# Squared-relu attention and a gated feed-forward: matmuls over all 128 rows replaced by pairs over 64 rows, in steps of two tiles

## The chip, the cores and the metric

The kernel runs on one core of a Trainium2 chip (trn2). The metric is device time in microseconds (us) of one execution, as the median of several. The engines are called by their short names: PE (TensorE, matmuls; PEld are its weight loads), DVE (VectorE), ACT (ScalarE), POOL (GpSimd) and SP (SyncE, which issues the DMAs). SBUF is the on-chip memory that all of them read, PSUM the eight banks that PE writes.

## The reference

Four batches of 3136 positions go through an attention without softmax and then a gated feed-forward with a convolution of three taps over positions. Inputs and outputs are float32.

```python
scores = (1 / S) * (z @ z.T)                 # S = 3136, z is 3136 x 64
x = u * (np.maximum(scores, 0) ** 2 @ v)     # u and v are 3136 x 256
h = np.maximum(x @ w_in, 0)                  # 3136 x 1024
conv = sum(conv_w[k] * shifted(h, k - 1) for k in range(3))
out = (h / (1 + np.exp(-conv))) @ w_out      # 3136 x 256
```

## The kernel before

Everything is held transposed, so that positions of a query lie along the free axis. The work is cut into 28 **blocks** of 448 query positions, seven to a batch. For each block the keys are walked in 25 **tiles** of 128 rows (the last has 64). Matmul operands are float32r; to keep precision each operand is split by ACT and DVE (or POOL) into a rounded part (`_hi`) and a remainder (`_lo`), and a product is the sum of three matmuls: hi by lo, hi by hi and lo by hi. A matmul takes weights of 128 rows by 128 columns and streams 448 columns (450 in the block that closes a batch).

For a tile `j` of block `n` the steps are these:

- `scores` (PE, L276 to L291): two matmuls into one bank of `ps_s`. z has only 64 features, so hi and lo parts lie one above the other in the 128 rows of `z_st`, and two matmuls give the whole product.
- ACT writes the scaled relu (`relu_s`, L422); DVE multiplies it by the scores in the bank (L563, `attn`), which gives the squared relu. For every two tiles ACT rounds (`attn_hi`, L417) and DVE takes the remainder (`attn_lo`, L551).
- `attend` (PE, L293 to L315): three matmuls for each of the two halves `c` of the 256 columns of v, into the two banks of `ps_av`.

After the last tile DVE multiplies `ps_av` by u (`x_sb`, L577). The feed-forward of block `n - 1` is done while block `n` is attended: for each of eight tiles `f` of the 1024 hidden columns `up` (six matmuls into `ps_h`), relu on ACT (`h_sb`, L454), first tap on ACT (L464), second and third on DVE (L590, L598), sigmoid on ACT (L470), the gate product on DVE (L604), rounding on ACT (`g_hi`, L476), the remainder on DVE (`g_lo`, L610, which raises `gated_split`), and for each pair `F` of hidden tiles `down` (twelve matmuls into `ps_y`, L345, which waits for `gated_split`).

Each engine has its own instruction queue, written in program order. A step of the loop is one tile: `scores` run `LEAD = 5` tiles ahead of `attend`, with three banks for scores. Two tables say in which step after its `up` each stage of the feed-forward is written on its engine:

```python
START = (3, 6, 10, 14)
STAGE = {"relu": 1, "tap0": 1, "tap1": 3, "tap2": 4, "gate": 5, "gated": 5, "round": 7, "split": 7, "down": 10}
```

So a split of pair `F` stands in step `START[F] + 7` and the `down` that reads it in step `START[F] + 10`, three tiles later. In the last block's feed-forward, with no attention beside it, other tables (`_ALONE`) hold. At the end of each batch ACT and POOL also round and split the next batch's z and v piece by piece (`z_st`, `v_hi`, `v_lo`).

## Time and profile before

| | |
|---|---|
| median of 3 runs | 1732.62 us (1732.59 to 1732.87) |
| profiled execution, its own time | 1733.34 us |
| its span, first to last instruction | 1731.6 us |
| PE busy | 1690.8 us (98%), 8232 matmuls and as many weight loads |
| DVE, ACT, POOL busy | 1370.7, 1217.3 and 196.0 us (79%, 70%, 11%) |
| share of the chain that ended last | PE 87%, DVE 5%, ACT 3% |
| mean granted PE clock | 0.996 |

The busy time of PE adds the time in which at least one matmul was under way; since one matmul is recorded for 0.36 us while the next starts 0.20 us later, it doesn't tell how close PE is to its rate. For that the distance from start to start is read from the timeline or from the counts in a window.

### The profile page before, as it was taken

The page shows a single profiled execution, that of the slowest core. Times are in us where ns is not written, and L with a number is a line of the kernel's source. Part 1 is how long each engine was busy: PE and PEld are TensorE (multiplying, and loading weights), DVE is VectorE, ACT ScalarE, POOL GpSimd, SP SyncE. Part 2 cuts the span into 40 slices and gives each one's busy share as a digit, 9 for nine tenths or more (in the row PEclk, how much of TensorE's full clock was granted, in tenths as well). Part 3 has the DMA queues.
Part 4 walks back from the last instruction along what each step waited for, and adds up shares of the span by engine and source line. Part 5 has one row for each costly group of instructions (what it writes and reads, how often), then busy time and mean ns, then how long its engine had stood idle before and what let it go on. Part 6 is the DMA issues. An engine that isn't in the chain of part 4 may idle for free.

```text
span 1731.6 us, 22661 instructions
## 1 busy us (share of the span) xinstructions
PE 1690.8 (98%) x8232; PEld 1551.4 (90%) x8232; DVE 1370.7 (79%) x1826; ACT 1217.3 (70%) x2022; POOL 196.0 (11%) x145
## 2 busy tenths in 40 slices
PE   8899999999999999999999999999999999999996
PEld 7799999988999999998899999999889999999995
DVE  6687778789877878788887788778888877878784
ACT  7667767777776777677777766767776776777664
POOL 6200000024000000003300000000420000000000
PEclk9999999999999999999999999999999999999998
DMA  5100000032000000003200000000310000000000
GB/s 148 53 27 1 27 27 1 27 91 77 1 27 27 1 28 27 27 1 106 62 1 28 27 28 1 27 28 11 108 50 27 1 27 28 3 25 27 22 1 21
DMA packets 28093, 55.34 MB, mean 32 GB/s; under 512 B 2896, under 2 KB 13648, under 8 KB 27984
## 3 DMA queue, kind: packets, MB, share of 16 engines
q1 hardware_dynamic: 27984, 53.90, 10.0%
q8 instruction: 66, 1.08, 0.2%
q14 instruction: 43, 0.35, 0.1%
HBM read 41.04 MB, written 12.85 MB: 31 GB/s over the span
## 4 chain that ended last, share of the span: by engine, by line
PE 87%; DVE 5%; ACT 3%; issue 1%; DMA 0%; POOL 0%; ACTq 0%; DVEq 0%; POOLq 0%
PE ps_y L345 15%; PE ps_h L332 14%; PE ps_av L308 14%; PE ps_av L307 14%; PE ps_av L309 14%; PE ps_s L290 7%; PE ps_s L289 7%; DVE g_sb L590 1%; DVE g_sb L598 1%; DVE g_lo L610 1%; DVE attn_lo L551 1%; ACT attn_hi L417 1%; PE ps_av L312 1%; PE ps_av L311 1%; DMA w_raw<-w_all 0%
## 5 line engine op out<-in xcount | busy, mean ns | idle before, releaser
L563 DVE SCALAR_TENSOR_TENSOR attn<-ps_s,relu_s 128x448 f32<-128x448 f32 x672 | 411.6, 617 | 231.2 <-ACT relu_s L422 230.5
L307 PE MATMUL ps_av<-attn_lo,v_hi 128*128 128x448 f32 x1344 | 493.1, 367 | 9.3 <-DVE attn_lo L551 7.1
L308 PE MATMUL ps_av<-attn_hi,v_hi 128*128 128x448 f32 x1344 | 493.4, 367 | 0.0
L309 PE MATMUL ps_av<-attn_hi,v_lo 128*128 128x448 f32 x1344 | 492.2, 366 | 0.0
L422 ACT ACTIVATE relu_s<-ps_s 128x448 f32<-128x448 f32 x672 | 357.9, 538 | 144.4 <-PE ps_s L290 144.2
L551 DVE TENSOR_TENSOR attn_lo<-attn,attn_hi 128x896 fp32r<-128x896 f32 x336 | 372.3, 1108 | 44.8 <-ACT attn_hi L417 44.8
L417 ACT ACTIVATE attn_hi<-attn 128x896 fp32r<-128x896 f32 x336 | 320.1, 953 | 97.4 <-DVE attn L563 94.4
L307 PEld LDWEIGHTS ps_av<-attn_lo,v_hi 128*128 128x128 f32 x1344 | 253.3, 188 | 34.4 <-issue 13.2
L308 PEld LDWEIGHTS ps_av<-attn_hi,v_hi 128*128 128x128 f32 x1344 | 253.2, 188 | 21.2
L309 PEld LDWEIGHTS ps_av<-attn_hi,v_lo 128*128 128x128 f32 x1344 | 253.0, 188 | 21.2
L289 PE MATMUL ps_s<-z_mv,z_st 128*128 128x448 f32 x672 | 247.0, 368 | 8.2 <-DVE z_st L656 6.5
L290 PE MATMUL ps_s<-z_mv,z_st 128*128 128x448 f32 x672 | 247.6, 368 | 0.0
L681 POOL TENSOR_TENSOR z_mv<-z_raw,z_mv 64x448 fp32r<-64x448 f32 x54 | 67.3, 1247 | 1208.3 <-ACT z_mv L382 1206.1
L610 DVE TENSOR_TENSOR g_lo<-g_sb,g_hi 128x896 fp32r<-128x896 f32 (+1 forms) x112 | 141.6, 1264 | 44.8 <-ACT g_hi L476 44.8
L345 PE MATMUL ps_y<-g_hi,w_hi 128*128 128x448 f32 (+1 forms) x448 | 164.5, 367 | 8.5 <-DVE g_lo L610 8.5
L332 PE MATMUL ps_h<-x_hi,w_hi 128*128 128x448 f32 x440 | 160.7, 365 | 10.8 <-ACT h_sb L454 7.8
L590 DVE SCALAR_TENSOR_TENSOR g_sb<-h_sb,taps,g_sb 128x448 f32<-128x448 f32 (+1 forms) x224 | 161.8, 761 | 7.0 <-ACT g_sb L464 6.9
L345 PE MATMUL ps_y<-g_lo,w_hi 128*128 128x448 f32 (+1 forms) x448 | 165.2, 369 | 0.0
L345 PE MATMUL ps_y<-g_hi,w_lo 128*128 128x448 f32 (+1 forms) x448 | 164.4, 367 | 0.0
L332 PE MATMUL ps_h<-x_hi,w_lo 128*128 128x448 f32 x440 | 162.5, 369 | 0.0
L332 PE MATMUL ps_h<-x_lo,w_hi 128*128 128x448 f32 x440 | 160.6, 365 | 0.0
L464 ACT ACTIVATE g_sb<-h_sb,taps 128x448 f32<-128x448 f32 (+1 forms) x224 | 149.7, 668 | 0.6
(56 smaller groups left out, 1883.0 us busy)
## 6 DMA issues: line engine op xcount, KB each, us to landing
u_sb<-u_win SPq DMA_DIRECT2D x28, 448.0 KB, 4.2
raw<-v_all SPq DMA_DIRECT2D x48, 256.0 KB, 2.6
out<-y_sb SPq DMA_DIRECT2D x24, 448.0 KB, 4.0
z_raw<-z_win SPq DMA_DIRECT2D x28, 224.0 KB, 4.2
raw<-z_all SPq DMA_DIRECT2D x24, 256.0 KB, 2.7
w_raw<-w_all SPq DMA_DIRECT2D x8, 256.0 KB, 2.7
out<-y_sb SPq DMA_DIRECT2D x4, 450.0 KB, 3.3
raw<-v_all SPq DMA_DIRECT2D x4, 128.0 KB, 2.4
```

The lines of the kernel that those rows point to most:

```text
L289: mm(scores_bank(j), w, z_mv[:, n % 2, 1, :], start=True, stop=False)
L290: mm(scores_bank(j), w, z_mv[:, n % 2, 0, :], start=False, stop=True).then_inc(scores_ready, 1)
L307: mm(acc, vh, lo, start=j == 0, stop=False)
L308: mm(acc, vh, hi, start=False, stop=False)
L309: done = mm(acc, vl, hi, start=False, stop=False)
L332: done = mm(h_bank(f, alone), w[:, at:at + P], x[:, c, :], start=k == 0, stop=k == 3 * CM - 1)
L345: done = mm(ps_y[:, c, 0:outputs(m)], w[:, at:at + P], g[:, e, 0:outputs(m)], start=F == 0 and e == 0 and k == 0, stop=F == FP - 1 and e = ...
L417: act.activation(attn_hi[:, q % 3, :, :], attn[:, q % 3, :, :], ACT.Copy).then_inc(attn_rounded, 1)
L422: act.activation(relu_slot(j), scores_bank(j), ACT.Relu, scale=1.0 / SEQ / SEQ).then_inc(relu_ready, 1)
L551: dve.tensor_tensor(attn_lo[:, q % 3, :, :], attn[:, q % 3, :, :], attn_hi[:, q % 3, :, :].bitcast(F32), ALU.subtract).then_inc(attn_split, 1)
L563: dve.scalar_tensor_tensor(dst, scores_bank(j), 0.0, relu_slot(j), ALU.max, ALU.mult).then_inc(attn_ready, 1)
L590: dve.scalar_tensor_tensor(g, h_sb[:, f, HALO:HALO + outputs(m)], taps[:, 1, f:f + 1], g, ALU.mult, ALU.add).then_inc(tap1_ready, 1)
```

## The change

Every matmul that took 128 rows becomes two of 64 rows, one with the weights and the moving operand of rows 0 to 63 (`UPPER`) and one with those of rows 64 to 127 (`LOWER`), written one behind the other in PE's queue. The two write different banks. A product over 128 rows into one bank is now a sum of an upper and a lower matmul that come at different times: in the first half of `attend` the upper rows go to bank `turn` and the lower rows to the other, and in the second half it is the other way round. The second half waits for a semaphore (`attn_turned`, `up_turned`, `down_turned`) that the last two matmuls of the first half raise. The last block's feed-forward keeps matmuls over 128 rows.

The scores of two tiles lie side by side: tile `2p` in the upper and tile `2p + 1` in the lower 64 rows of `z_hi` and `z_lo`, three pairs of matmuls for two tiles in two banks. The last tile of 64 keys is held in both halves and takes three pairs in `attend`.

A step is now a pair of tiles, 13 to a block. Scores run `AHEAD = 3` pairs ahead, with two banks for scores, and `ps_h` has two banks. ACT writes the relu straight into `attn` and DVE multiplies it in place. The feed-forward has new tables by step; the last `down` of a block (`F = 3`) is done in step 0 of the block after the next. Window splits of z are now over 128 rows. The number of DMAs and their sizes hardly change.

```diff
-LEAD = 5
-SBANKS = 3
+AHEAD = 3
...
-START = (3, 6, 10, 14)
-STAGE = {"relu": 1, "tap0": 1, "tap1": 3, "tap2": 4, "gate": 5, "gated": 5, "round": 7, "split": 7, "down": 10}
...
+UP_FIRST = {1: 0, 3: 1, 5: 2}
+UP_SECOND = {2: 0, 4: 1, 6: 2}
+DOWN_FIRST = {7: 0, 9: 1, 11: 2}
+DOWN_SECOND = {8: 0, 10: 1, 12: 2}
+UP_FIRST_END = {7: 3}
+UP_SECOND_END = {8: 3}
+RELU_AT = {3: 0, 5: 1, 7: 2, 9: 3}
+TAP01_AT = {4: 0, 6: 1, 8: 2, 10: 3}
+GATE_AT = {5: 0, 7: 1, 9: 2, 11: 3}
+SPLIT_AT = {6: 0, 8: 1, 10: 2, 12: 3}
+WINDOW_AT = 6
...
-            def scores(n, b, j, first):
...
-                if j == LAST:
-                    if not first:
-                        pe.wait_ge(h_ready, n * FT)
-                elif j >= SBANKS or not first:
-                    pe.wait_ge(attn_ready, n * STEPS + j - SBANKS + (1 if j >= SBANKS else 0))
-                w = z_st[:, j * P:(j + 1) * P]
-                mm(scores_bank(j), w, z_mv[:, n % 2, 1, :], start=True, stop=False)
-                mm(scores_bank(j), w, z_mv[:, n % 2, 0, :], start=False, stop=True
-                   ).then_inc(scores_ready, 1)
-
-            def attend(n, b, j, first):
-
-                if j % VTILES == 0:
-                    pe.wait_ge(piece_split, b * NP + AT["v", j // VTILES] + 1)
-                    pe.wait_ge(attn_split, n * ROUNDS + j // 2 + 1)
+            def scores(n, p):
...
+                    pe.wait_ge(attn_ready, n * TILES + 2 * p)
+                at = p * P
+                for k, (w, z) in enumerate(((z_hi, 1), (z_lo, 0), (z_hi, 0))):
+                    for e in members(p):
+                        rows = (UPPER, LOWER)[e]
+                        done = mm(ps_s[:, e, 0:BLOCK], w[rows, at:at + P], z_mv[rows, n % 2, z, :],
+                                  start=k == 0, stop=k == 2)
+                        if k == 2:
+                            done.then_inc(scores_ready, 1)
...
+            def attend(n, p, second):
+
+                if second:
+                    pe.wait_ge(attn_turned, 2 * (n * LAST + p) + 2)
+                else:
+                    pe.wait_ge(piece_split, place(batch_of(n), "v", p) + 1)
+                    pe.wait_ge(attn_split, n * PAIRS + p + 1)
+                    if p == 0 and n > 0:
+                        pe.wait_ge(x_ready, n * CM)
+                turn = (p + int(second)) % 2
+                for e in members(p):
+                    j = 2 * p + e
+                    for k, (v, a) in enumerate(((v_hi, attn_lo), (v_hi, attn_hi), (v_lo, attn_hi))):
+                        for rows, c in ((UPPER, turn), (LOWER, 1 - turn)):
+                            done = mm(ps_av[:, c, 0:BLOCK], v[rows, j * MODEL + c * P:j * MODEL + (c + 1) * P],
+                                      a[rows, 2 * slot(n, p) + e, :],
+                                      start=p == 0 and not second and e == 0 and k == 0, stop=p == LAST and k == 2)
+                            if e == members(p)[-1] and k == 2:
+                                done.then_inc(attn_used if second or p == LAST else attn_turned, 1)
...
-                    if j == 0 and not first:
...
-                    vh = v_hi[:, j * MODEL + c * P:j * MODEL + (c + 1) * P]
-                    vl = v_lo[:, j * MODEL + c * P:j * MODEL + (c + 1) * P]
-                    acc = ps_av[:, c, 0:WIDE]
-                    if j < LAST:
-                        hi = attn_hi[:, j // 2 % 3, j % 2, :]
-                        lo = attn_lo[:, j // 2 % 3, j % 2, :]
-                        mm(acc, vh, lo, start=j == 0, stop=False)
-                        mm(acc, vh, hi, start=False, stop=False)
-                        done = mm(acc, vl, hi, start=False, stop=False)
-                    else:
-                        mm(acc, vh, attn_last_parts[:, :], start=False, stop=False)
-                        done = mm(acc, vl, attn_last_parts[:, :], start=False, stop=True)
...
+            def down_half(m, F, second):
...
+                if second:
+                    pe.wait_ge(down_turned, 2 * (m * FP + F) + 2)
+                else:
+                    pe.wait_ge(gated_split, m * FP + F + 1)
+                    if m + F > 0:
+                        pe.wait_ge(down_done, 2 * (m * FP + F))
+                turn = int(second)
+                for e in range(2):
+                    for k, (w, g) in enumerate(((w_hi, g_hi), (w_hi, g_lo), (w_lo, g_hi))):
+                        for rows, c in ((UPPER, turn), (LOWER, 1 - turn)):
+                            at = CM * FF + (2 * F + e) * MODEL + c * P
+                            done = mm(ps_y[:, c, 0:outputs(m)], w[rows, at:at + P], g[rows, e, 0:outputs(m)],
+                                      start=F == 0 and e == 0 and k == 0 and not second,
+                                      stop=F == FP - 1 and e == 1 and k == 2 and second)
+                            if e == 1 and k == 2:
+                                done.then_inc(down_done if second else down_turned, 1)
...
-                done.then_inc(down_done, 1)
...
+            def middle(n, p):
+
+                m = n - 1
...
+                if n > 0 and p in UP_FIRST:
+                    up_half(m, UP_FIRST[p], False)
+                if n > 0 and p in UP_SECOND:
+                    up_half(m, UP_SECOND[p], True)
+                if n > 0 and p in DOWN_FIRST:
+                    down_half(m, DOWN_FIRST[p], False)
+                if n > 0 and p in DOWN_SECOND:
+                    down_half(m, DOWN_SECOND[p], True)
...
+            def end(n, p):
...
+                if n > 0 and p in UP_FIRST_END:
+                    up_half(m, UP_FIRST_END[p], False)
+                if n > 0 and p in UP_SECOND_END:
+                    up_half(m, UP_SECOND_END[p], True)
+
...
+                for p in range(PAIRS):
+                    if p == LAST:
+                        attend(n, p, False)
+                        middle(n, p)
+                    else:
+                        attend(n, p, False)
+                        middle(n, p)
+                    if ahead_of(n, p, AHEAD):
+                        scores(*ahead_of(n, p, AHEAD))
+                    if p < LAST:
+                        attend(n, p, True)
+                    end(n, p)
...
-            for j in range(LEAD):
-                scores(0, 0, j, True)
-            for n in range(BLOCKS):
-                for t in range(STEPS):
-                    if t + LEAD < STEPS:
-                        scores(n, batch_of(n), t + LEAD, n == 0)
-                        attend(n, batch_of(n), t, n == 0)
...
-                        attend(n, batch_of(n), t, n == 0)
-                        if n + 1 < BLOCKS:
-                            scores(n + 1, batch_of(n + 1), t + LEAD - STEPS, False)
-                    if n > 0:
-                        feed_forward(n - 1, t, False)
...
-            def attention(n, j, first):
-
-                act.wait_ge(scores_ready, n * STEPS + j + 1)
-                act.activation(relu_slot(j), scores_bank(j), ACT.Relu,
-                               scale=1.0 / SEQ / SEQ).then_inc(relu_ready, 1)
-                for back, q in rounds_after(j, ROUND_LAG):
-                    if not (first and back):
-                        round_attn(n - back, q, first)
...
+            def relu_scores(n, p):
+
+                for e in members(p):
+                    act.wait_ge(scores_ready, tiles_through(n, p))
+                    if n * PAIRS + p >= 3:
+                        act.wait_ge(attn_split, pair_before(n, p, 3) + 1)
+                    act.activation(attn[:, slot(n, p), e, :], ps_s[:, e, 0:BLOCK], ACT.Relu, scale=1.0 / SEQ / SEQ
+                                   ).then_inc(relu_ready, 1)
...
+            def step(n, p):
+                m = n - 1
+                if n > 0 and p in GATE_AT:
+                    convolve_last(m, GATE_AT[p])
+                if ahead_of(n, p, AHEAD - 1):
+                    split_attn(*ahead_of(n, p, AHEAD - 1))
+                if n > 0 and p == 0:
+                    split_x(m)
+                if p == LAST:
+                    gate_by_u(n)
+                if ahead_of(n, p, AHEAD):
+                    multiply(*ahead_of(n, p, AHEAD))
+                if n > 0 and p in TAP01_AT:
+                    convolve(m, TAP01_AT[p])
+                if n > 0 and p in GATE_AT:
+                    apply_gate(m, GATE_AT[p])
+                if n > 0 and p in SPLIT_AT:
+                    split_gated(m, SPLIT_AT[p])
```

The functions that aren't shown here (`up_half`, the order of ACT's `step`, the loading of pieces) follow the same pattern; the tables at the top say in which step each of their calls stands.

Three places show what moves. The first is DVE's queue in the feed-forward. Before, around the split `g_lo` (L610) of one pair of hidden tiles:

```order
L551 TENSOR_TENSOR attn_lo<-attn,attn_hi 128x896 [waits attn_rounded]
L604 TENSOR_TENSOR g_sb<-h_sb,g_sb 128x2x448 [waits gate_ready]
L563 SCALAR_TENSOR_TENSOR attn<-ps_s,relu_s 128x448 [waits relu_ready]
L563 SCALAR_TENSOR_TENSOR attn<-ps_s,relu_s 128x448 [waits attn_split,relu_ready]
L551 TENSOR_TENSOR attn_lo<-attn,attn_hi 128x896 [waits attn_rounded]
L610 TENSOR_TENSOR g_lo<-g_sb,g_hi 128x2x448 [waits gated_rounded]
```

After, in step 10 and the start of step 11 (L614 is the product of scores and relu, L644 and L652 the second and third tap, L664 the split `g_lo`):

```order
L621 TENSOR_TENSOR attn_lo<-attn,attn_hi 128x896 [waits attn_rounded]
L614 SCALAR_TENSOR_TENSOR attn<-ps_s,attn 128x448 [waits relu_ready] x2
L644 SCALAR_TENSOR_TENSOR g_sb<-h_sb,taps,g_sb 128x448 [waits tap0_ready] x2
L664 TENSOR_TENSOR g_lo<-g_sb,g_hi 128x2x448 [waits gated_rounded]
L652 SCALAR_TENSOR_TENSOR g_sb<-h_sb,taps,g_sb 128x448 [waits tap1_ready] x2
```

In both the split stands behind two products of scores. After the change both products belong to one pair of tiles whose scores are written in the same step, and two second taps stand between them and the split.

The second is PE's queue ahead of the `down` that reads such a split. Before:

```order
L307 MATMUL ps_av<-attn_lo,v_hi 128x448 [waits attn_split,piece_split]
L308 MATMUL ps_av<-attn_hi,v_hi 128x448
L309 MATMUL ps_av<-attn_hi,v_lo 128x448
L307 MATMUL ps_av<-attn_lo,v_hi 128x448
L308 MATMUL ps_av<-attn_hi,v_hi 128x448
L309 MATMUL ps_av<-attn_hi,v_lo 128x448
L289 MATMUL ps_s<-z_mv,z_st 128x448 [waits attn_ready,piece_split,z_split]
L290 MATMUL ps_s<-z_mv,z_st 128x448
L345 MATMUL ps_y<-g_hi,w_hi 128x448 [waits gated_split]
```

After, from the last pair of the second half of `attend` in step 10 on (a row with x2 is one pair; the first pair of each part stands as two rows or as one with its wait and one without):

```order
L317 MATMUL ps_av<-attn_hi,v_lo 128x448 x2
L317 MATMUL ps_av<-attn_lo,v_hi 128x448 [waits attn_split,piece_split]
L317 MATMUL ps_av<-attn_lo,v_hi 128x448
L317 MATMUL ps_av<-attn_hi,v_hi 128x448 x2
L317 MATMUL ps_av<-attn_hi,v_lo 128x448 x2
L317 MATMUL ps_av<-attn_lo,v_hi 128x448 x2
L317 MATMUL ps_av<-attn_hi,v_hi 128x448 x2
L317 MATMUL ps_av<-attn_hi,v_lo 128x448 x2
L358 MATMUL ps_y<-g_hi,w_hi 128x448 [waits down_done,gated_split]
```

After the change the only matmuls between the scores of step 10 and this `down` are the two halves of `attend`, of six pairs each; the split stands in DVE's queue of step 10, and the `down` in the middle of step 11. Before, the split stands three tiles ahead of its `down`.

The third is the border between two blocks on DVE, before and after (x_sb is the product of `ps_av` and u that frees the two banks for the next block):

```order
L551 TENSOR_TENSOR attn_lo<-attn,attn_hi 128x896 [waits attn_rounded]
L563 SCALAR_TENSOR_TENSOR attn<-ps_s,relu_s 128x448 [waits relu_ready]
L577 TENSOR_TENSOR x_sb<-ps_av,u_sb 128x448 [waits first_half_ready,u_loaded]
L577 TENSOR_TENSOR x_sb<-ps_av,u_sb 128x448 [waits attn_used]
L563 SCALAR_TENSOR_TENSOR attn<-ps_s,relu_s 128x448 [waits attn_split,relu_ready]
L551 TENSOR_TENSOR attn_lo<-attn,attn_hi 128x896 [waits attn_rounded]
L563 SCALAR_TENSOR_TENSOR attn<-ps_s,relu_s 128x448 [waits relu_ready]
```

```order
L621 TENSOR_TENSOR attn_lo<-attn,attn_hi 128x896 [waits attn_rounded]
L629 TENSOR_TENSOR x_sb<-ps_av,u_sb 128x448 [waits attn_used,u_loaded]
L629 TENSOR_TENSOR x_sb<-ps_av,u_sb 128x448
L614 SCALAR_TENSOR_TENSOR attn<-ps_s,attn 128x448 [waits relu_ready] x2
L664 TENSOR_TENSOR g_lo<-g_sb,g_hi 128x2x448 [waits gated_rounded]
```

After the change x_sb stands behind the split `attn_lo` of the pair whose scores were written one step earlier, in both its parts, and `attend` of the next block waits for both.

## Rows read from the trace of the kernel before

**Rows 1.** The page: busy times and instructions of the engines.

```profile
PE 1690.8 (98%) x8232; PEld 1551.4 (90%) x8232; DVE 1370.7 (79%) x1826; ACT 1217.3 (70%) x2022; POOL 196.0 (11%) x145
```

**Rows 2.** Windows: length, busy us (x instructions) of PE, PEld, DVE, ACT, POOL; clock, DMA.

```profile
0.00:68.00 68.00, 54.48 (x234) 48.14 (x235) 43.80 (x57) 48.00 (x82) 42.85 (x33) 0.97 0.43 128
68.00:1683.00 1615.00, 1604.00 (x7872) 1476.08 (x7871) 1303.33 (x1741) 1148.32 (x1908) 153.19 (x112) 1.00 0.09 28
1300.00:1600.00 300.00, 300.00 (x1478) 277.15 (x1477) 239.40 (x329) 210.54 (x347) 11.82 (x10) 1.00 0.06 20
1683.00:1731.60 48.60, 32.29 (x130) 27.19 (x128) 23.56 (x30) 20.93 (x32) 0.00 (x0) 0.89 0.05 19
```

**Rows 3.** The longest wait of PE on another engine: total us, times, longest.

```profile
PE ps_y L345 <- DVE g_lo L610: 8.5, 6, 2.5
```

**Rows 4.** Timeline, PE matmuls and weight load: start us, lasting us.

```profile
600.33 0.37 PE L290 MATMUL ps_s<-z_mv,z_st 128*128 128x448 f32 x1
600.33 0.19 PEld L307 LDWEIGHTS ps_av<-attn_lo,v_hi 128*128 128x128 f32 x1
600.54 0.36 PE L307 MATMUL ps_av<-attn_lo,v_hi 128*128 128x448 f32 x1
```

**Rows 5.** Timeline after a wait of PE, then at half clock.

```profile
1702.02 0.19 PEld L332 LDWEIGHTS ps_h<-x_hi,w_hi 128*128 128x128 f32 x1 [2.86 <-ACT h_sb L454]
1702.13 0.19 PEld L332 LDWEIGHTS ps_h<-x_lo,w_hi 128*128 128x128 f32 x1
...
1707.79 0.58 PE L345 MATMUL ps_y<-g_hi,w_hi 128*128 128x450 f32 x1
1708.16 0.58 PE L345 MATMUL ps_y<-g_lo,w_hi 128*128 128x450 f32 x1
```

**Rows 6.** Timeline: scores, relu and product.

```profile
603.16 0.36 PE L290 MATMUL ps_s<-z_mv,z_st 128*128 128x448 f32 x1
603.56 0.54 ACT L422 ACTIVATE relu_s<-ps_s 128x448 f32<-128x448 f32 x1 [0.67 <-PE ps_s L290]
...
607.66 0.97 ACT L422 ACTIVATE relu_s<-ps_s 128x448 f32<-128x448 f32 x2
...
614.43 0.54 ACT L422 ACTIVATE relu_s<-ps_s 128x448 f32<-128x448 f32 x1
615.00 0.62 DVE L563 SCALAR_TENSOR_TENSOR attn<-ps_s,relu_s 128x448 f32<-128x448 f32 x1 [0.98 <-ACT relu_s L422]
```

**Rows 7.** Timeline of DVE in a later stretch.

```profile
627.47 0.62 DVE L563 SCALAR_TENSOR_TENSOR attn<-ps_s,relu_s 128x448 f32<-128x448 f32 x1
628.00 1.08 DVE L551 TENSOR_TENSOR attn_lo<-attn,attn_hi 128x896 fp32r<-128x896 f32 x1
629.00 1.27 DVE L590 SCALAR_TENSOR_TENSOR g_sb<-h_sb,taps,g_sb 128x448 f32<-128x448 f32 x2
630.19 0.61 DVE L563 SCALAR_TENSOR_TENSOR attn<-ps_s,relu_s 128x448 f32<-128x448 f32 x1
...
635.45 1.15 DVE L563 SCALAR_TENSOR_TENSOR attn<-ps_s,relu_s 128x448 f32<-128x448 f32 x2
```

**Rows 8.** Timeline: the end of a split and the matmul it releases.

```profile
1705.64 1.09 DVE L610 TENSOR_TENSOR g_lo<-g_sb,g_hi 128x900 fp32r<-128x900 f32 x1
1706.78 0.47 PE L345 MATMUL ps_y<-g_hi,w_hi 128*128 128x450 f32 x1 [2.05 <-DVE g_lo L610]
```

**Rows 9.** Timeline: an earlier split, x_sb, and the matmul of the split.

```profile
600.53 1.09 DVE L610 TENSOR_TENSOR g_lo<-g_sb,g_hi 128x896 fp32r<-128x896 f32 x1 [0.21 <-ACT g_hi L476]
603.36 0.37 PE L345 MATMUL ps_y<-g_hi,w_hi 128*128 128x448 f32 x1
603.70 1.14 DVE L577 TENSOR_TENSOR x_sb<-ps_av,u_sb 128x448 f32<-128x448 f32 x2
```

**Rows 10.** Groups of instructions by line: busy us, mean ns.

```profile
L417 ACT ACTIVATE attn_hi<-attn 128x896 fp32r<-128x896 f32 x336 | 320.1, 953 | 97.4 <-DVE attn L563 94.4
L395 ACT ACTIVATE v_hi<-raw 128x512 fp32r<-128x512 f32 x48 | 30.1, 627 | 0.0
```

596 lines of the change are left out of this document (291 added, 305 removed).

## The prediction

> **What bounds the kernel now.** I read the page first: PE is busy for 98% of the span, DVE for 79%, ACT for 70% [rows 1]. Then windows over the whole span, to see where PE is not fed [rows 2]. The waits of PE on other engines are short and few; the first in the list has 8.5 us in all [rows 3]. In the timeline a matmul starts 0.20 to 0.21 us after the one before [rows 4]. The window from 1300 to 1600 us has PE busy throughout with 1478 matmuls, 0.2030 us each, and I use that as one **slot**. 8232 slots are 1671 us. The other 60 us of the span are 68 - 234 x 0.203 = 20.5 at the start, 48.6 - 130 x 0.203 = 22.2 at the end and 1615 - 7872 x 0.203 = 17 between [rows 1, 2]. So two things can change the time: the number and length of slots, and new waits of PE.
>
> A slot is 448 columns, which at 2.4 GHz would take 187 ns. At half clock the distance is 0.375 us [rows 5], and 448 columns at 1.2 GHz are 373 ns. So only at full clock some 16 ns lie between two matmuls. The weight load of the next one starts with the matmul now running [rows 4] and lasts 0.19 us; after a wait the second load starts 0.11 us after the first [rows 5].
>
> **Slots.** Attention has per block 24 tiles of 6 matmuls and 4 for the last: 148; now 12 steps of 12 pairs and 3: 147 pairs. Scores: 50, now 12 x 3 + 3 = 39 pairs. Feed-forward: 96 and 96. So 294 slots of one matmul become 282 slots of one pair, over 28 blocks 8232 become 7896 (48 of the last block's stay single, and so do 12 of the block before). If a pair takes the time of one matmul before, that saves 336 x 0.203 = 68 us.
>
> What does a pair take? No row shows one. From below: both halves stream 448 columns at the same time and the 16 ns vanish since one half streams while the other changes weights: 187 to 189 ns. From above, if they run one after the other: 2 x 0.203 = 406 ns. Between: each half behaves as the whole array did, 203 ns; or the two weight loads follow one another at the 0.11 us of rows 5: 216 ns. I take 203 ns, the row of the same operand sizes at the same clock.
>
> On this the Trainium skill has two rules. "TensorE: Matmul & The Clock Gate", section "LDWEIGHTS (loading the stationary operand)", gives columns / 1.2, so 107 ns whatever the rows are; the 0.11 us of rows 5 agree. Two loads a pair would by that be 213 ns, which is the rival below. The same page, "The mechanism" of its part on packing, says a weight load overlaps a running matmul only when the row group differs. By that a slot before would be 187 + 107 = 294 ns; the trace has 0.203 with the load inside it [rows 4], so the measurement decides, and the gain that this rule would promise (an estimate: 294 - 189 = 105 ns in each slot) isn't to be had by hiding loads that are hidden already.
>
> **The new waits.** DVE and ACT have the work they had: relu, product, rounding and split per tile, in 13 larger steps (the split of the last tile is now over 128 rows; POOL's window splits too, and POOL is idle for 89%). What changes is distance. In the feed-forward `down` waits for a split (`g_lo`) which stands in DVE's queue of the step before, behind the product of that step's scores. Count from T, the start of the last scores matmul of that step (T of step 10 for the `down` in step 11):
>
> - first relu starts 0.40 later, lasts 0.54; the product starts 0.03 after it: T + 0.97 [rows 6]. The second relu is over at T + 1.37, in time [rows 6].
> - two products last 1.15, and DVE's next instruction starts some 0.08 before the last ends [rows 7]: T + 2.04.
> - two second taps: the next starts 1.19 later [rows 7]: T + 3.23.
> - the split, 1.09; 0.05 until PE's weight load [rows 8], 0.11 until the matmul streams [rows 5]: T + 4.48.
>
> PE has until then the scores matmul itself and two halves of `attend`, 13 slots = 2.64 us. It waits **1.84 us**, in step 7 and in step 11. In step 9 the second half of the last `up` (six slots) stands between as well: 19 slots = 3.86, a wait of 0.62. Before, the split ended at 601.62 and its `down` came at 603.36 with PE never idle [rows 9].
>
> At the border of two blocks `attend` waits for both x_sb. DVE does them behind the split `attn_lo` of the pair scored in step 11. From T of step 11: second product over at T + 2.12, rounding 0.95 on ACT with 0.03 on each side [rows 10]: T + 3.13, split 1.00 to the next start [rows 7], two x_sb 1.14 [rows 9], 0.16 to PE: T + 5.43. PE has 1 + 6 + 3 + 6 + 3 = 19 slots = 3.86: wait **1.57 us**. Call the end of x_sb X; `attend` starts at X + 0.16. DVE's two products start at X - 0.08 and X + 0.45, the split of the last pair at X + 0.98, and its `down` can stream at X + 0.98 + 1.09 + 0.16 = X + 2.23. PE is there after six slots, at X + 1.38: wait **0.85 us**. Queued behind each wait of PE are the next scores, for which ACT and DVE wait in turn, so DVE's idle time doesn't help to catch up: its queue starts again only from those scores.
>
> Sum per block: 1.84 + 0.62 + 1.84 + 1.57 + 0.85 = 6.7 us, against 12 slots less = 2.4 us. It occurs in 26 blocks (block 0 has no feed-forward, the last one's is done alone): 175 us. In the three blocks that close a batch ACT also rounds a piece of v in nearly every step (0.63, [rows 10]) ahead of the relu of `up`, which makes that 0.5 to 0.9 late three times: some 7 us.
>
> **Sum.** 7896 x 0.203 = 1603; start, end and small waits as before 60; new waits 175 + 7; 1733.3 - 1731.6 = 1.7 outside the span. Together **1847 us** for a profiled execution like the one before (1733.3; the median of the runs shown is 1732.6, 0.7 lower). I forecast 1847, 6.6% slower. A change of 0.2% is about what a measurement of this kernel tells from none.
>
> **Rivals.**
> - *Pairs at 187 to 189 ns.* For it: the 16 ns are missing at half clock, so they are no work of the array [rows 5]; with two halves one could stream on while the other turns. Against: each half still turns after each of its matmuls. 7896 x 0.189 = 1492. But PE then has less to do ahead of each wait: 13 slots are 0.19 shorter, 19 slots 0.27, six 0.09, and about 0.15 each shows up in steps 3 and 5 at the relu of `up`: 8.0 per block, 208, and 8. 1492 + 60 + 216 + 2 = 1770. Chance 0.25.
> - *Weight loads in a row, 216 ns.* Each pair has two loads of 0.11 [rows 5]. 7896 x 0.216 = 1706; waits shrink to 5.9 per block, 153 and 5: 1706 + 60 + 158 + 2 = 1926. Chance 0.17.
> - *Pairs don't run together at all.* Then 7896 x 0.406 = 3206, and 13 slots (5.3 us) cover every chain above: 3206 + 60 + 2 = 3268. Against: the halves share neither rows nor bank. Chance 0.05.
> - *Faster.* It is one mechanism, a shorter way from scores to the split, and needs the 187 ns too: 7896 x 0.187 + 60 + 2 = 1539 leaves 194 us for waits, 7.2 per block beside 7 in the closing ones, where at 187 ns I count 8.1. If a matmul over 64 rows leaves the array sooner than the 0.40 of rows 6, each of five chains shortens by up to 0.2: 7.1 per block, 1539 + 185 + 7 = 1731; with the product, done in place now, 0.05 shorter each time as well it would be about 1718. It decides from 7.2 us per block down. At 203 ns it would take waits of 2.5 per block, which no row lets me see. Chance 0.08.
> - *As forecast, 203 ns and waits of 6 to 7.5 per block:* 1828 to 1868, chance 0.45.
>
> **Range.** From the case at 189 ns downwards with a little shorter chains to the case at 216 ns: 1755 to 1935 leaves out the serial case (0.05), the faster one (0.08) and the far ends of the others (0.07). Chances: faster by over 0.2% 0.09, within 0.2% 0.03, slower 0.88.
>
> **What would show it.** The distance from one pair to the next in an undisturbed stretch of the timeline gives the slot: near 203, 189, 216 or 406 ns. In the list of waits PE on the split `g_lo` should come first with four waits in a block, 1.8 the typical long one and some 130 us in all, then PE on x_sb with 27 times 1.6. The release of `down` should come 4.5 us after the last scores of the step before. DVE and ACT should be busy for the same us and a lower share. The prediction is wrong if a pair is off the 203 ns by more than 10, or if PE's waits per block are outside 6 to 7.5 us, for instance because the granted clock falls in the new waits; at 1683 to 1731 us with 40% idle it was still 0.89 [rows 2].

## The result, and the profile after

The median of the changed kernel is **1934.18 us**, that of the kernel before measured beside it 1732.71 us: a ratio of 1.1162, 95% interval 1.1140 to 1.1184. One of its four executions took 7328 us, and no trace of it was kept; the other three lie between 1933.73 and 1934.43. The profiled execution has a span of 1932.1 us. The forecast was 1847 us with a range of 1755 to 1935. So the direction was right and the time lies at the very edge of the range, 87 us above the value; most of this document is about those 87 us.

The page answers to [rows 1]; its row of clocks has the granted clock in 40 slices, in tenths of full speed:

```profile
PE 1710.3 (89%) x15600; PEld 1539.1 (80%) x15600; DVE 1379.7 (71%) x1825; ACT 1188.2 (61%) x2010; POOL 133.2 (7%) x106
...
PEclk9999999998998999899999999989999999999998
```

The windows answer to [rows 2]:

```profile
68.00:1883.00 1815.00, 1628.82 (x15047) 1471.00 (x15045) 1313.23 (x1740) 1120.83 (x1901) 101.43 (x77) 0.96 0.08 25
1300.00:1600.00 300.00, 266.20 (x2486) 240.73 (x2484) 220.20 (x288) 190.31 (x327) 29.73 (x22) 0.97 0.10 30
```

DVE and ACT do the same work as before to within 3%, at a lower share. PE is no longer busy throughout. And the clock has eights in the middle of the kernel and 0.96 as its mean there, where before it was 1.00.

The list of waits, engine by engine (total us, times, longest), answers to [rows 3]:

```profile
PE ps_y L358 <- DVE g_lo L664: 141.8, 103, 3.5
PE ps_av L317 <- DVE x_sb L629: 42.2, 27, 2.7
PE ps_s L298 <- DVE attn L614: 12.1, 12, 2.5
```

The first two are the two that were forecast, in that order: `down` on the split, and `attend` on x_sb at the border of two blocks. Together 184.0 us. A length in this list runs from the recorded end of the matmul before, which is recorded for 0.36 us though the next could start after 0.20; so it leaves out 0.16 us of each wait, and the 0.11 us behind it. How the 184 compare with the forecast's 182 is told further down.

The timeline of an undisturbed stretch answers to [rows 4] (a row with x2 that lasts 0.36 us is a pair that starts together):

```profile
652.57 0.36 PE L317 MATMUL ps_av<-attn_hi,v_hi 64*128 64x448 f32 x2
652.77 0.36 PE L317 MATMUL ps_av<-attn_hi,v_lo 64*128 64x448 f32 x2
652.97 0.36 PE L339 MATMUL ps_h<-x_hi,w_hi 64*128 64x448 f32 x2
653.17 0.36 PE L339 MATMUL ps_h<-x_lo,w_hi 64*128 64x448 f32 x2
```

A pair runs together and the next comes 0.20 us later; the mean over the 6865 undisturbed distances in the records is 0.2010 us. The weight loads of both halves lie beside the running matmuls:

```profile
600.05 0.55 PE L317 MATMUL ps_av<-attn_hi,v_hi 64*128 64x448 f32 x2
600.05 0.18 PEld L317 LDWEIGHTS ps_av<-attn_hi,v_lo 64*128 64x128 f32 x1
600.05 0.18 PEld L317 LDWEIGHTS ps_av<-attn_hi,v_hi 64*128 64x128 f32 x1
600.25 0.55 PE L317 MATMUL ps_av<-attn_hi,v_lo 64*128 64x448 f32 x2
```

Both start together at 600.05, so two loads of 64 rows do not follow one another at 0.11 us. They belong to two different products: here the halves are not in step, the lower one is a slot behind the upper, and a row with x2 that lasts 0.55 us holds two matmuls 0.20 us apart. That is so for some 7 us in most blocks, in which a `down` of one half runs beside scores of the other (680 starts in the whole trace).

The chain from scores to the `down` of step 11 or 7, in the timeline of all engines (it answers to [rows 6 to 8]):

```profile
599.64 0.36 PE L298 MATMUL ps_s<-z_mv,z_hi 64*128 64x448 f32 x1
600.08 0.98 ACT L473 ACTIVATE attn<-ps_s 128x448 f32<-128x448 f32 x2 [1.29 <-PE ps_s L298]
600.66 1.16 DVE L614 SCALAR_TENSOR_TENSOR attn<-ps_s,attn 128x448 f32<-128x448 f32 x2 [1.21 <-ACT attn L473]
601.73 1.27 DVE L644 SCALAR_TENSOR_TENSOR g_sb<-h_sb,taps,g_sb 128x448 f32<-128x448 f32 x2
602.92 1.08 DVE L664 TENSOR_TENSOR g_lo<-g_sb,g_hi 128x896 fp32r<-128x896 f32 x1
604.05 0.56 PE L358 MATMUL ps_y<-g_hi,w_hi 64*128 64x448 f32 x2 [1.65 <-DVE g_lo L664]
```

From the last scores at 599.64 to the matmul of `down` at 604.05 plus the 0.11 until it streams it is 4.5 us, as forecast. In step 6 of a block the same chain is longer. There POOL splits a part of the next block's z (L724), and it runs beside the second taps:

```profile
646.55 1.15 POOL L724 TENSOR_TENSOR z_mv<-z_raw,z_mv 128x448 fp32r<-128x448 f32 x1 [67.93 <-ACT z_mv L445]
646.69 2.09 DVE L644 SCALAR_TENSOR_TENSOR g_sb<-h_sb,taps,g_sb 128x448 f32<-128x448 f32 x2
649.84 0.47 PE L358 MATMUL ps_y<-g_hi,w_hi 64*128 64x448 f32 x2 [2.47 <-DVE g_lo L664]
```

The two taps last 2.09 us and not 1.27. The first of them takes 1.49 us beside the POOL instruction (1.47 to 1.49 in 23 of the 26 blocks), where the 183 taps with nothing on POOL take 0.68. The split, and with it the `down` of step 7, is 0.8 us later: the wait is 2.47 us and not 1.65. The forecast had 1.84 for both.

The wait of step 11 one block later shows what else was not in the sum:

```profile
671.76 0.47 PE L358 MATMUL ps_y<-g_hi,w_hi 64*128 64x448 f32 x2 [1.65 <-DVE g_lo L664]
672.08 0.36 PE L358 MATMUL ps_y<-g_lo,w_hi 64*128 64x448 f32 x2
672.28 0.36 PE L358 MATMUL ps_y<-g_hi,w_lo 64*128 64x448 f32 x2
672.47 0.50 PE L358 MATMUL ps_y<-g_hi,w_hi 64*128 64x448 f32 x2
672.77 0.58 PE L358 MATMUL ps_y<-g_lo,w_hi 64*128 64x448 f32 x2
673.14 0.58 PE L358 MATMUL ps_y<-g_hi,w_lo 64*128 64x448 f32 x2
673.51 0.58 PE L298 MATMUL ps_s<-z_mv,z_hi 64*128 64x448 f32 x2
```

The window of 4 us behind it, with the clock as its third value from the end:

```profile
672.00:676.00 4.00, 4.00 (x26) 3.59 (x26) 2.42 (x4) 1.10 (x3) 0.00 (x0) 0.57 0.00 0
```

The wait ends at 671.76, the next pairs start 0.32, 0.20 and 0.19 us apart, and after one more of 0.30 the distance is 0.37 us: PE is at the lower of its two levels, 1.2 GHz. The granted clock is 0.57 in this window. Since there are two levels, a mean clock c over a span S means 2 x (1 - c) x S at the lower one: 2 x 0.044 x 1932 = 170 us, against 2 x 0.004 x 1732 = 14 us before. A pair takes 0.373 there and not 0.201, so each us at the lower level loses 1 - 0.201 / 0.373 = 0.46 us where PE has work: 156 x 0.46 = 72 us at most.

### The profile page after: what moved, and what is told of

Same layout as the page of the kernel before. It is cut to its first block, busy times and chain, and to the rows that moved or that the text cites. A ratio compares the mean times of both kernels' runs of the same rounds, so it can differ in the third digit from the quotient of the medians.

```text
span 1932.1 us, 37660 instructions
## 1 busy us (share of the span) xinstructions
PE 1710.3 (89%) x15600; PEld 1539.1 (80%) x15600; DVE 1379.7 (71%) x1825; ACT 1188.2 (61%) x2010; POOL 133.2 (7%) x106
## 4 chain that ended last, share of the span: by engine, by line
PE 59%; DVE 27%; ACT 8%; issue 4%; DMA 1%; POOL 0%; ACTq 0%; SPq 0%
PE ps_av L317 24%; PE ps_y L358 14%; PE ps_s L298 10%; PE ps_h L339 10%; DVE attn L614 7%; DVE g_sb L644 7%; DVE g_lo L664 6%; DVE attn_lo L621 4%; ACT attn L473 3%; ACT attn_hi L482 2%; DVE x_sb L629 2%; ACT g_sb L516 1%; DVE g_sb L658 1%; ACT g_sb L522 1%; DVE g_sb L652 1%
## 5 line engine op out<-in xcount | busy, mean ns | idle before, releaser
L473 ACT ACTIVATE attn<-ps_s 128x448 f32<-128x448 f32 x700 | 344.8, 543 | 622.8 <-PE ps_s L298 595.2
L317 PE MATMUL ps_av<-attn_lo,v_hi 64*128 64x448 f32 x2744 | 563.8, 370 | 42.2 <-DVE x_sb L629 42.2
L614 DVE SCALAR_TENSOR_TENSOR attn<-ps_s,attn 128x448 f32<-128x448 f32 x700 | 404.9, 618 | 262.2 <-ACT attn L473 261.5
L621 DVE TENSOR_TENSOR attn_lo<-attn,attn_hi 128x896 fp32r<-128x896 f32 (+1 forms) x364 | 392.8, 1079 | 251.5 <-ACT attn_hi L482 250.4
L317 PE MATMUL ps_av<-attn_hi,v_hi 64*128 64x448 f32 x2744 | 558.7, 366 | 0.0
L317 PE MATMUL ps_av<-attn_hi,v_lo 64*128 64x448 f32 x2744 | 557.1, 365 | 0.0
L317 PEld LDWEIGHTS ps_av<-attn_lo,v_hi 64*128 64x128 f32 x2744 | 308.2, 189 | 71.7 <-issue 52.0
L482 ACT ACTIVATE attn_hi<-attn 128x896 fp32r<-128x896 f32 (+1 forms) x364 | 335.1, 921 | 27.5 <-DVE attn L614 25.3
L317 PEld LDWEIGHTS ps_av<-attn_hi,v_hi 64*128 64x128 f32 x2744 | 308.6, 189 | 17.7
L358 PE MATMUL ps_y<-g_hi,w_hi 64*128 64x448 f32 (+1 forms) x856 | 194.0, 414 | 141.8 <-DVE g_lo L664 141.8
L317 PEld LDWEIGHTS ps_av<-attn_hi,v_lo 64*128 64x128 f32 x2744 | 306.4, 188 | 15.6
L298 PE MATMUL ps_s<-z_mv,z_hi 64*128 64x448 f32 x1400 | 294.4, 387 | 17.6 <-DVE attn L614 12.1
L358 PE MATMUL ps_y<-g_lo,w_hi 64*128 64x448 f32 (+1 forms) x856 | 184.0, 391 | 0.0
L644 DVE SCALAR_TENSOR_TENSOR g_sb<-h_sb,taps,g_sb 128x448 f32<-128x448 f32 (+1 forms) x224 | 170.6, 801 | 9.3 <-ACT g_sb L516 9.3
L652 DVE SCALAR_TENSOR_TENSOR g_sb<-h_sb,taps,g_sb 128x448 f32<-128x448 f32 (+1 forms) x224 | 145.8, 691 | 0.0
```

The lines of the kernel that those rows point to most:

```text
L298: done = mm(ps_s[:, e, 0:BLOCK], w[rows, at:at + P], z_mv[rows, n % 2, z, :], start=k == 0, stop=k == 2)
L317: done = mm(ps_av[:, c, 0:BLOCK], v[rows, j * MODEL + c * P:j * MODEL + (c + 1) * P], a[rows, 2 * slot(n, p) + e, :], start=p == 0 and not ...
L358: done = mm(ps_y[:, c, 0:outputs(m)], w[rows, at:at + P], g[rows, e, 0:outputs(m)], start=F == 0 and e == 0 and k == 0 and not second, sto ...
L473: act.activation(attn[:, slot(n, p), e, :], ps_s[:, e, 0:BLOCK], ACT.Relu, scale=1.0 / SEQ / SEQ).then_inc(relu_ready, 1)
L482: act.activation(attn_hi[:, at:at + k, :], attn[:, slot(n, p), 0:k, :], ACT.Copy).then_inc(attn_rounded, 1)
L614: dve.scalar_tensor_tensor(a, ps_s[:, e, 0:BLOCK], 0.0, a, ALU.max, ALU.mult).then_inc(attn_ready, 1)
```

## The experiments

What was to be told apart: whether the waits are the chain in the order of the queues (my theory) or something in the matmuls; whether the missing 87 us are the granted clock; whether 64-row pairs bring that clock, or cost or gain anything themselves.

All kernels compute the whole output. "g_lo" and "x_sb" are the totals of PE's waits on the two, "low" is 2 x (1 - clock) x span, good to some 2 us since the clock is rounded. (Before, e7 and e10 have the last block's own `down` in their "g_lo"; in the others it is a line of its own, of some 8 us, and left out.) Where a text below says "by the distances", the distances from one slot to the next are added up over the whole trace: what they have above the undisturbed 0.201 us (0.203 in before, e7 and e10) is put down to waits if PE stood still ahead of that slot or of the one before it, to the clock if it falls into a stretch at the lower level, and else to small delays. Each group was measured beside its own runs of the kernel before: e1 to e4 at 1733.28 us, e5 and e7 to e9 at 1732.51, e10 and e11 at 1733.84 (there is no e6).

| | median us | ratio, 95% interval | span | clock | low | g_lo | x_sb |
|---|---|---|---|---|---|---|---|
| before | 1732.71 | | 1731.6 | 0.996 | 14 | 8.5 | 2.1 |
| after | 1934.18 | 1.1162 (1.1140 to 1.1184) | 1932.1 | 0.956 | 170 | 141.8 | 42.2 |
| e1 | 1772.48 | 1.0229 (1.0214 to 1.0244) | 1770.2 | 0.970 | 106 | 2.1 | 66.3 |
| e2 | 2016.10 | 1.1637 (1.1619 to 1.1654) | 2014.9 | 0.976 | 97 | 132.8 | 26.0 |
| e3 | 1836.54 | 1.0599 (1.0581 to 1.0616) | 1834.9 | 0.992 | 29 | 0 | 38.0 |
| e4 | 1727.64 | 0.9973 (0.9962 to 0.9984) | 1723.7 | 0.992 | 28 | 12.4 | 35.8 |
| e5 | 1836.27 | 1.0599 (1.0583 to 1.0615) | 1834.8 | 0.976 | 88 | 53.8 | 57.5 |
| e7 | 1830.05 | 1.0567 (1.0551 to 1.0582) | 1826.6 | 0.992 | 29 | 75.4 | 8.9 |
| e8 | 1878.09 | 1.0841 (1.0823 to 1.0859) | 1876.4 | 0.993 | 26 | 66.6 | 26.0 |
| e9 | 1732.76 | 1.0002 (0.9992 to 1.0011) | 1732.1 | 0.988 | 42 | 2.1 | 35.6 |
| e10 | 2162.06 | 1.2467 (1.2450 to 1.2484) | 2160.6 | 0.944 | 242 | 300.5 | 13.7 |
| e11 | 1729.49 | 0.9972 (0.9963 to 0.9981) | 1727.0 | 0.990 | 35 | 12.3 | 35.5 |

### e1: rounding and split of the gated values ahead of the step's scores

In ACT's step the rounding moves ahead of the relu of the scores, in DVE's step the split ahead of their product.

```diff
+                if n > 0 and p in SPLIT_AT:
+                    round_gated(m, SPLIT_AT[p])
...
-                if n > 0 and p in SPLIT_AT:
-                    round_gated(m, SPLIT_AT[p])
...
+                if n > 0 and p in SPLIT_AT:
+                    split_gated(m, SPLIT_AT[p])
                 if ahead_of(n, p, AHEAD):
                     multiply(*ahead_of(n, p, AHEAD))
...
-                if n > 0 and p in SPLIT_AT:
-                    split_gated(m, SPLIT_AT[p])
```

> The changed kernel with the rounding and the split of the gated pair (g_hi on ACT, g_lo on DVE) written ahead of the relus and products of their step instead of behind them; all matmuls as in the changed kernel. Theory A (the time is lost in PE's waits on g_lo, and the half-clock stretches follow those waits): no wait of PE on g_lo is left in the steady blocks, one of about 2.6 us per block on x_sb stays, the clock comes back to 0.98 or more, and the time is 1587 (7896 pairs of 0.201) + 60 + 26 x 2.7 + 2 = about 1720, with some half-clock stretches behind the x_sb wait up to 1745. Theory B (matmuls over 64 rows keep the clock down or are slower in themselves, and the waits matter little): the granted clock stays near 0.956 and the time above 1850.

Measured: 1772.48 us, 162 us less than after, with the same matmuls in the same order on PE. The wait on g_lo is gone (from 141.8 to 2.1 us), so it was the place of the rounding and the split in the queues. By the distances 135 us came back in waits and 31 by the clock, and 5 were lost in small delays. The size was missed by 27 us at least and the clock is 0.970, not 0.98 or more: the wait on x_sb has grown, to 2.39 us in 23 blocks, and behind 19 of these 23 a stretch at half clock begins within 1.6 us; behind the other four none does. Timeline of PE:

```profile
681.08 0.52 PE L317 MATMUL ps_av<-attn_lo,v_hi 64*128 64x448 f32 x2 [2.40 <-DVE x_sb L629]
681.37 0.61 PE L317 MATMUL ps_av<-attn_hi,v_hi 64*128 64x448 f32 x2
681.72 0.63 PE L317 MATMUL ps_av<-attn_hi,v_lo 64*128 64x448 f32 x2
```

### e5: only DVE's half of that edit

ACT's rounding stays behind the relu.

```diff
+                if n > 0 and p in SPLIT_AT:
+                    split_gated(m, SPLIT_AT[p])
                 if ahead_of(n, p, AHEAD):
                     multiply(*ahead_of(n, p, AHEAD))
```

> The changed kernel with DVE's half of the first experiment's edit alone: the split `g_lo` stands ahead of the product of the step's scores, while ACT's rounding `g_hi` stays behind the relu of those scores. Theory (the wait of `down` is the chain scores, relu, product, taps, split in the order of the queues): the split now starts when ACT's `g_hi` is done, near T + 1.4 + 1.1 = 2.5 us and ends near T + 3.6 and not T + 4.5, so each long wait of `down` gets 0.9 us shorter, 2.3 us a block, 60 us, and a part of the half clock goes too: 1840 to 1885 us. Rival (product and `attn_lo` get later by what the split waits for ACT, so that the wait moves to `attend` or to the relu): 1915 to 1950, with PE on attn_lo among the first of the list of waits.

Measured: 1836.27, 98 us less than after, a little below the lower end of what the theory said. The list of waits of PE:

```profile
PE ps_av L317 <- DVE x_sb L629: 57.5, 24, 2.4
PE ps_y L358 <- DVE g_lo L664: 53.8, 53, 1.3
PE ps_s L298 <- DVE attn L614: 23.2, 40, 2.7
```

The longest wait of `down` is down from 3.5 to 1.3 us. By the distances 59 us came back in waits and 38 by the clock. What the rival named is there too, but small: PE on attn_lo is not in the list, but scores wait for the later product, 23.2 us in place of 12.1, and `attend` for x_sb, 57.5 in place of 42.2. So DVE's place is worth 98 of the 162 us of e1, and ACT's rounding on top of it the other 64.

### e8: work without effect in place of the waits

PE adds zeros (`fill`) to `ps_av` behind the first half of `attend` in steps 7 and 11, and to `ps_y` ahead of `attend` in step 0.

```diff
+FILL = {7: 7, 11: 7}
+FILL_BORDER = 4
...
+                    for k in range(FILL[p]):
+                        for rows, c in ((UPPER, turn), (LOWER, 1 - turn)):
+                            done = mm(ps_av[:, c, 0:BLOCK], w_hi[rows, c * P:(c + 1) * P], fill[rows, :],
+                                      start=False, stop=False)
...
+                for k in range(FILL_BORDER):
+                    for rows, c in ((UPPER, 0), (LOWER, 1)):
+                        mm(ps_y[:, c, 0:BLOCK], w_hi[rows, c * P:(c + 1) * P], fill[rows, :],
+                           start=False, stop=False)
```

In those two steps the last of these matmuls raises `attn_turned`.

> The changed kernel, in which PE does work without effect in the time in which it would wait: seven pairs that add zeros to ps_av ahead of the first half of `down` in steps 7 and 11, and four pairs that add zeros to ps_y ahead of `attend` at the border of two blocks. 18 pairs are 3.6 us a block, laid into waits of 1.8 to 2.9, 1.8 to 2.9 and 1.0 to 2.7 us. Theory (the 172.7 us at half clock come from PE standing still for 1.8 to 2.9 us at a time, and cost some 78 us): the waits that are left are 0.4 to 1.5 us, the clock is 0.985 or more, and the time goes DOWN to 1855 to 1880 us although PE does 468 pairs more. Rival 1 (the clock falls for another reason, the form of the matmuls or the mean load over a block): still 100 us or more at half clock and 1932 to 1960 us. Rival 2 (the half clock costs little, since a slow PE only uses up waits that follow): the clock is up but the time stays at 1925 to 1940.

This is the direct test of the clock: PE does 16564 matmuls and not 15600, 482 pairs or 97 us more, and the queues of DVE and ACT are as they were, but for one memset at the start. The page and PE's waits:

```profile
PE 1744.9 (93%) x16564; PEld 1572.8 (84%) x16564; DVE 1379.6 (74%) x1826; ACT 1187.1 (63%) x2010; POOL 134.1 (7%) x106
```

```profile
PE ps_y L377 <- DVE g_lo L686: 66.6, 104, 2.1
PE ps_av L329 <- DVE x_sb L651: 26.0, 27, 2.1
```

The window that stands above for after:

```profile
1300.00:1600.00 300.00, 281.11 (x2698) 253.49 (x2696) 222.86 (x291) 191.26 (x325) 28.68 (x21) 0.99 0.09 31
```

The time fell to 1878.09 us, 56 us less than after, though PE does more. Fill and waits that are left are 97 + 93 = 190 us, as much as the 184 us of waits of after: the chain is as long as it was. What changed is the clock, 0.993 in place of 0.956. By the distances PE's slots are 98 us more, its waits 89 us less, and the clock gives back 65 us, which makes the 56.

The second rival is out by the time. Of the first, the form of the matmuls is out, since it is the same. The mean load over a block is not out by e8 alone, since the zeros raise it too; e1 and e3 settle it. Slots times their distance are 0.90 of the span both in e8 (clock 0.993) and in e1 (0.970), and in e3 they are 0.86 with 0.992. The clock does not go with the mean load. It goes with single waits: in e1 there is one of 2.4 us in nearly every block, in e3 and e8 most have 1.2 and less.

### e7 and e10: the same waits in the kernel before, with whole matmuls

The kernel before with one number changed, 8 in e7 and 7 in e10:

```diff
-STAGE = {"relu": 1, "tap0": 1, "tap1": 3, "tap2": 4, "gate": 5, "gated": 5, "round": 7, "split": 7, "down": 10}
+STAGE = {"relu": 1, "tap0": 1, "tap1": 3, "tap2": 4, "gate": 5, "gated": 5, "round": 7, "split": 7, "down": 7}
```

> The kernel before with one number changed: `down` stands 8 steps behind its `up` and not 10, so that whole 128-row matmuls wait for the split `g_lo` as the pairs do in the changed kernel. By the rows of before the split ends 1.74 us ahead of its `down`; two steps are 16 slots of 0.203 (22 for the second pair F, where an `up` lies between), 3.25 and 4.5 us, so PE should wait 1.5 us three times and 2.7 us once in a block, 7.2 us, 26 times: 187 us. Theory (the half clock follows the waits, whatever the matmuls are): stretches of 3.4 us at half clock in most blocks, behind the 2.7 us wait above all, 26 to 50 of them, worth 45 to 85 us more: 1965 to 2005 us and a mean granted clock under 0.97. Rival (the half clock belongs to 64-row matmuls, and whole ones keep the clock through such waits, as before does at 0.996): 1915 to 1925 us, clock 0.99 or more.

e7 missed both expectations, and told nothing of the rival: the waits came to 75.4 us and not 187. There are three in a block, of 0.5 to 1.0 us; the slack is larger than at the one place, [rows 9], from which I had taken it. By the distances the waits cost 92 us more than before and the clock 4, which is nearly all of the 95 us between the spans; the clock is 0.992.

> The kernel before with `down` 7 steps behind its `up`, in the very step of its split. With 8 steps PE, on whole 128-row matmuls, had waits of 0.5 to 1.0 us behind g_lo (75.4 us in 87), and the granted clock stayed at 0.992. One step less takes away 8 slots three times in a block and 14 once, 1.62 and 2.84 us, 7.7 in a block, and as the waits have used up the slack these come on top of the waits: 2.1 to 3.8 us each, 26 x 7.7 = 200 us more than 1830. Theory (half clock follows standstills of some 2 us and more, whatever the matmuls are): one to four stretches of 3.4 us at half clock in every block, 90 to 300 us in all, 45 to 150 us of time: 2070 to 2170 us, clock 0.93 to 0.975. Rival (whole matmuls keep the clock): 2015 to 2040 us, clock 0.985 or more, and the half clock in the changed kernel would come with 64-row matmuls.

e10 decides between the two. The timeline of PE:

```profile
638.90 0.47 PE L345 MATMUL ps_y<-g_hi,w_hi 128*128 128x448 f32 x1 [3.30 <-DVE g_lo L610]
639.21 0.37 PE L345 MATMUL ps_y<-g_lo,w_hi 128*128 128x448 f32 x1
...
640.51 0.57 PE L345 MATMUL ps_y<-g_lo,w_hi 128*128 128x448 f32 x1
640.89 0.57 PE L345 MATMUL ps_y<-g_hi,w_lo 128*128 128x448 f32 x1
```

The window there, and the first of the list of waits:

```profile
640.00:650.00 10.00, 10.00 (x43) 9.12 (x43) 4.95 (x8) 4.49 (x9) 0.00 (x0) 0.83 0.01 2
```

```profile
PE ps_y L345 <- DVE g_lo L610: 300.5, 111, 5.8
```

Whole 128-row matmuls fall to 0.37 us from start to start behind a wait just as pairs do, and the mean clock is 0.944, lower than that of after. 2162 us lies in the theory's range (2070 to 2170). By the distances the waits cost 325 us more than before, the clock 103 and the slots 2, which is the 429 us between the spans. The price taken from the clock alone gives the same 103: 228 us more at the lower level, x 0.454. The waits themselves came out larger than expected, 225 us more than in e7 in the list and not 200.

### e2 and e3: matmuls over 128 rows again, but for the scores

In the changed kernel (e2) and in e1 (e3) all of `attend` but the last tile, `up` and `down` become whole matmuls again, two tiles a step and all waits in place. Scores stay in pairs. The core of the edit in `down_half`; `attend` and `up_half` are alike:

```diff
-                        for rows, c in ((UPPER, turn), (LOWER, 1 - turn)):
-                            at = CM * FF + (2 * F + e) * MODEL + c * P
-                            done = mm(ps_y[:, c, 0:outputs(m)], w[rows, at:at + P], g[rows, e, 0:outputs(m)],
...
+                        c = turn
+                        at = CM * FF + (2 * F + e) * MODEL + c * P
+                        done = mm(ps_y[:, c, 0:outputs(m)], w[:, at:at + P], g[:, e, 0:outputs(m)],
```

> The changed kernel's queues, steps, waits and banks, but attend (save the last tile), up and down take whole matmuls over 128 rows again, six in the first half for one bank and six in the second half for the other; the scores stay pairs over 64 rows. Theory A: nearly nothing changes against the changed kernel, 1934 plus 6804 x 0.002 us for a slot of 0.203 in place of 0.201, less a little shorter waits: 1935 to 1950, granted clock 0.95 to 0.96. Theory B: the clock rises to 0.99 and the time falls to about 1855. If going from pairs to whole matmuls and back (twice in a step, 728 times) costs something of its own, the time is above 1950, 0.1 us at each turn giving some 70 us, and the timeline shows it at the scores.

> Both edits together: early rounding and split, and whole matmuls over 128 rows in attend, up and down. Theory A: against the run with the early split alone this shows what the pairs are worth where PE hardly waits: 6804 slots of 0.203 in place of 0.201 give 10 to 15 us more, so about 1735 to 1760, clock 0.98 or more. Theory B: clearly faster than the run with the early split alone. Turns between pairs and whole matmuls would come on top here as well.

The slot is the same for both forms: whole matmuls start 0.2005 us apart in e2 and e3, pairs 0.2010 in after. Yet both kernels are slower than their partners, by 82 and 64 us. The timeline of e3 where form and form meet:

```profile
621.18 0.36 PE L365 MATMUL ps_y<-g_lo,w_hi 128*128 128x448 f32 x1
621.38 0.37 PE L365 MATMUL ps_y<-g_hi,w_lo 128*128 128x448 f32 x1
621.67 0.47 PE L298 MATMUL ps_s<-z_mv,z_hi 64*128 64x448 f32 x2
621.98 0.36 PE L298 MATMUL ps_s<-z_mv,z_lo 64*128 64x448 f32 x2
622.18 0.37 PE L298 MATMUL ps_s<-z_mv,z_hi 64*128 64x448 f32 x2
622.48 0.47 PE L318 MATMUL ps_av<-attn_lo,v_hi 128*128 128x448 f32 x1
622.79 0.37 PE L318 MATMUL ps_av<-attn_hi,v_hi 128*128 128x448 f32 x1
```

And its weight loads there:

```profile
621.67 0.18 PEld L298 LDWEIGHTS ps_s<-z_mv,z_hi 64*128 64x128 f32 x2 [0.30 <-issue]
621.78 0.19 PEld L298 LDWEIGHTS ps_s<-z_mv,z_lo 64*128 64x128 f32 x2
```

Elsewhere a load starts with the running matmul. Here it starts only at 621.67, after 0.30 us in which PEld stood still, and the second one 0.11 later, as after a wait in [rows 5]. So a turn from one form to the other costs 0.09 to 0.10 us at the turn and 0.11 at the next matmul, 0.20 together (means over 737 undisturbed turns: 0.297 and 0.309 in place of twice 0.201). The Trainium skill says in "TensorEngine Tiling (Array Packing)", section "Key Properties", that a change of the tiling mode drains TensorE; it gives no price. The trace agrees, and puts it at 0.20 us here. There are 777 turns, some of them at a wait or in a stretch at half clock; the undisturbed ones, 706 in e2 and 738 in e3, come to 145 and 152 us. As a check by the times: e3's span is 111.2 us longer than that of e4, which has the same clock. By the distances it has the 152 us of turns more, 28 us less in waits, 5 less in slots and 8 less in small delays: 111. e2 was expected at 1935 to 1950 us, or above 1950 with some 70 us if turns cost 0.1 us; the turns are there, at twice that price.

This also sets apart the clock: e3 has 29 us at the lower level and e1 106, with the same queues on DVE and ACT. PE comes later to each wait, the wait is shorter (38.0 us in all and not 66.3; 1.16 and not 2.39 in most blocks), and the clock stays. e3 has another form of matmul too, so by itself it doesn't part the two; e8 and e10 do.

### e4, e11 and e9: the version that is faster than before

e4 is e1 with x_sb ahead of the split and of the last tile's work on DVE:

```diff
+                if p == LAST:
+                    gate_by_u(n)
                 if ahead_of(n, p, AHEAD - 1):
                     split_attn(*ahead_of(n, p, AHEAD - 1))
...
-                if p == LAST:
-                    gate_by_u(n)
```

> The early split, and DVE also takes the two x_sb products ahead of the attn_lo split in the last step of a block. Theory A: the wait on x_sb falls from 2.6 to about 1.5 us and 0.85 us of wait for the last down comes back: 1 us a block less at most if each wait counts by its length, so 5 to 10 us below the early split alone, about 1712 to 1735; more if shorter waits leave the clock up. If it is below 1729 it beats the kernel before. Theory B: no change against the early split alone.

It gave 45 us less than e1 and not 5 to 10. The wait on x_sb is 30.5 us less in all and 1.28 in a typical block, and that on g_lo 10 us more, so the list gives 20. By the distances the waits give only 13, since e4 has 84 waits and e1 61 and each costs 0.27 us more than its length in the list, and the clock gives 33: together the 46.5 us between the spans. The wait in the border of a block, and the window:

```profile
662.22 0.47 PE L317 MATMUL ps_av<-attn_lo,v_hi 64*128 64x448 f32 x2 [1.28 <-DVE x_sb L629]
```

```profile
1300.00:1600.00 300.00, 291.45 (x2845) 266.93 (x2843) 239.06 (x331) 210.12 (x353) 6.95 (x6) 1.00 0.06 21
```

> The version with splits, roundings and x_sb earlier once more, the same file, against more runs of the kernel before, since 0.9973 lies near the 0.2% that a measurement can tell. If it is faster: ratio 0.9965 to 0.9980, 1726 to 1730 us. If the first comparison was luck: 0.999 to 1.001.

The second comparison gave 0.9972 (0.9963 to 0.9981): this version is 0.28% faster than the kernel before, little but twice the same. (The profiled execution of e4, at 1725.52 us, is among its fastest; its eight lie between 1725.47 and 1731.25.)

> The version that was faster than before (splits, roundings and x_sb earlier) with two more moves: the last `down` of a block one step later in each half, and in step 12 rounding and split of the gated values behind relu and product again, so that nothing stands ahead of the last tile's scores. It should take away the wait of `down` in step 0 (12.4 us in 30 waits) and shorten x_sb's 35.8 us by up to 10. Theory: 1710 to 1724 us, 0.987 to 0.995 of before. Rival (x_sb's chain is set by scores, relu, product and `attn_lo` of the last pair alone): 1724 to 1732, no change against that version.

e9 lost it again: 1732.76. x_sb's wait stayed (35.6 us in 26), as the rival had it, and `scores` wait more, 27.5 us in 40 in place of 15.6 in 15, 0.5 us at the scores behind x_sb in most blocks. The wait of `down` in step 0 did go (from 12.4 to 2.1 us), and it did not pay. Two things were moved at once, and no run parts them; that the later place of rounding and split is what the scores wait for is argued, not shown.

## Why the prediction was right, and where it was short

The differences to the kernel before, in us, as forecast and by the distances of the two traces:

| | forecast | measured |
|---|---|---|
| slots | -68 | -85 |
| waits | +182 | +215 |
| clock | no term | +71 |
| small delays, start and end | 0 | -1 |
| together | +114 | +200 |
| time of the profiled execution | 1847 | 1933.9 |

- **Slots.** 7896 at 0.203 were forecast, 0.201 measured: some 16 us too much. That a half behaves as the whole array does was right; 187 to 189 ns did not appear, nor did loads in a row at 216 ns, nor a serial array.
- **The waits.** The mechanism was right: g_lo first, x_sb second, 27 times; 4.5 us from scores to `down` in step 11. e1 and e5 show the cause, the order on DVE and ACT. In size this term was 33 us short. The forecast counts a wait from when PE could start to when the matmul streams, which is 0.16 + 0.11 = 0.27 us more than the list of waits shows. Counted so, a block without a stretch at half clock has 2.74 in step 7, 0.71 in step 9, 1.92 in step 11, 1.87 on x_sb and 0.76 in step 0, 8.0 us, where 1.84, 0.62, 1.84, 1.57 and 0.85, 6.7 us, were forecast. The wrong step is that of step 7: the taps beside POOL's instruction take 0.8 us more, some 20 us in all. The forecast named POOL's window splits only as work for an engine with time to spare. By this count the waits are outside the 6 to 7.5 us per block that the forecast had named, so its own sign of being wrong did show. That the list's 184 us are so near to 182 is luck.
- **The clock.** **The largest part of the miss is the last step of the cost of the waits: each was priced at its own length, and the falling clock got no term.** The forecast named it among the things that would make it wrong, and left it out since in [rows 2] the last stretch had 0.89. The runs show the term: 156 us more at 1.2 GHz and, by the distances, 71 us of time. 65 us came back in e8 when the waits were filled, and e10, with 103 us, shows that it does not depend on pairs. The forecast looked for a falling clock in the length of the waits; it shows in the distances behind them.
- **Slips without weight.** 96 slots of the last block stay single and not 48, and PE is idle for a third of 1683 to 1731 us and not for 40%; neither changes the sum.
- **The rival "loads in a row", 1926 us,** was the nearest in time and wrong in mechanism. That the range held the result, 0.8 us from its end, is luck, since its upper end is owed to a case that did not occur.
- **The gain by fewer slots** is real: by the distances e4 has 85 us less in slots than before, and gives nearly all of it back: 67 in waits, 6 by the clock, 5 in small delays.
- **What stays open.** Which waits bring a stretch at the lower level. A wait of 2.47 us at 649.84 in after did not, one of 1.65 at 671.76 did, and waits of 2.39 us in e1 did and did not, so length alone does not tell. It counts all the same: over all twelve traces 5 of 368 waits between 0.7 and 1.35 us have a stretch that begins in them or in the 2 us behind, in after 23 of 44 between 1.35 and 1.75 (in e2 none of 24), and in e10 57 of 60 over 2.55. Why whole matmuls start 0.2005 us apart in e2 and e3 and 0.2030 before.

## What to carry to other kernels

A new wait of PE costs its length in the list, here 0.27 us on top of it, and it may cost PE's clock behind it: in after waits of 0.4 to 3.5 us cost 215 us by themselves and 71 by the clock; in e4 and e7, where most are 1.3 us or less, the clock cost 6 and 4. So in a sum of waits the clock stands as a term of its own. What PE will wait for goes, on every engine of its chain, ahead of that step's work for which nobody waits yet (e1, e5). For each DVE instruction of such a chain it is worth a look at what POOL does beside it. Pairs over 64 rows gave nothing in themselves here, where weight loads were hidden already (0.201 us against 0.2005 for whole matmuls in e2); the gain is in the products with 64 rows, scores and the last tile, and mixing pairs with whole matmuls cost 0.20 us at each turn (e2, e3).

## What was not expected of the hardware

- A turn from 64-row to 128-row matmuls or back costs 0.20 us, in two parts, 0.10 at the turn and 0.11 at the next matmul (e3).
- Work without effect made the kernel faster: 97 us of zeros added to PSUM took 56 us off the time (e8).
- Two 64-row weight loads start together and last 0.18 us each, beside the running matmuls, and the two halves can run a slot or more out of step (after, 598 to 600 us).
- DVE is slower beside POOL, but not in every instruction. In after second taps (L644) that run beside a POOL instruction take 1.35 us in the mean, 0.68 otherwise, and six splits `g_lo` took 2.16 us and not 1.08; the 58 products that read PSUM (L614) beside POOL take 0.61 us as all others do.
